# Block sums multiplied and copied beside a pair's own first scores, exponentials signalled one by one, and four weight loads queued last, in an attention and two-MoE kernel

## The reference

```python
k_sum = k.reshape(B, H, nb, block, D).max(axis=3)
v_sum = v.reshape(B, H, nb, block, D).mean(axis=3)
scores_l = scale * np.matmul(q, k.transpose(0, 1, 3, 2))
scores_s = scale * np.einsum('bhsd,bhnd->bhsn', q, k_sum) + np.log(block)
scores_all = np.concatenate([np.where(mask_l, scores_l, -1e9), scores_s], axis=-1)
a = softmax(scores_all)
out = np.matmul(a, np.concatenate([v, v_sum], axis=2))
```

## Time and profile before

| | |
|---|---|
| median of 3 runs | 379.94 us (379.44 to 381.62) |
| the profiled execution, its own time | 379.92 us |
| its span, first to last instruction | 378.2 us |
| PE, DVE, ACT, POOL busy | 86%, 47%, 38%, 27% of the span |
| mean granted TensorE clock | 0.969 of full |
| attention, soft mixture, switch layer | to about 122, to about 199, to the end |

### The profile page before, as it was taken

How to read it: one execution, slowest core, us unless ns; L and a number is a source line. 1 busy time by engine, 2 the same in 40 slices (tenths; PEclk the granted TensorE clock), 3 DMA queues, 4 the chain that set the end, 5 groups by cost and what they waited for, 6 DMA issues and landing times.

```text
span 378.2 us, 9016 instructions
## 1 busy us (share of the span) xinstructions
PE 326.6 (86%) x3272; PEld 233.9 (62%) x3273; DVE 175.9 (47%) x406; ACT 143.6 (38%) x329; POOL 101.1 (27%) x181
## 2 busy tenths in 40 slices
PE   0879879889898999969877795999999999999991
PEld 0556656667677754232325264788888888888880
DVE  2577867877885553360116596132331323213231
ACT  1476666666876422310110262123232322313221
POOL 5665675676764000000000000121211212112121
PEclk9999999999999999987998999699999999999996
DMA  7999999999999716999942900110101111010110
GB/s 306 362 425 408 414 423 415 419 419 420 410 385 406 297 50 227 383 390 405 393 156 83 364 2 0 57 47 36 55 28 55 41 42 55 28 55 34 49 56 32
DMA packets 23851, 81.64 MB, mean 216 GB/s; under 512 B 2312, under 2 KB 2312, under 8 KB 21776
## 3 DMA queue, kind: packets, MB, share of 16 engines
q1 hardware_dynamic: 20640, 73.08, 49.1%
q0 software_dynamic: 1920, 6.29, 4.4%
q10 hardware_dynamic: 1264, 1.92, 1.5%
HBM read 74.99 MB, written 6.29 MB: 215 GB/s over the span
## 4 chain that ended last, share of the span: by engine, by line
PE 57%; DMA 16%; DVE 11%; ACT 4%; POOL 4%; issue 4%; SPq 2%; ACTq 0%; DVEq 0%; POOLq 0%
PE ps L904 33%; DMA ring<-in_vt 11%; DMA ring<-in_moe_w 5%; PE ps L630 3%; POOL ring L503 3%; PE ps L643 3%; PE ps L890 3%; PE ps L600 3%; ACT work L962 2%; PE ps L787 2%; SPq L285 2%; PE ps L746 2%; DVE ps L1128 2%; PE ps L651 1%; PE ps L709 1%
## 5 line engine op out<-in xcount | busy, mean ns | idle before, releaser
L904 PE MATMUL ps<-high_w2b,hid_high 128*128 (+1 forms) x184 | 73.1, 397 | 4.1 <-DVE hid_low L1372 4.1
L904 PE MATMUL ps<-low_w2b,hid_high 128*128 (+1 forms) x184 | 72.8, 396 | 0.0
L904 PE MATMUL ps<-high_w2b,hid_low 128*128 (+1 forms) x184 | 72.5, 394 | 0.0
L962 ACT ACTIVATE work<-ps,small 128x120 f32<-128x120 f32 x192 | 53.9, 368 | 39.3 <-DVE small L1132 39.1
L556 POOL DMA_INDIRECT out_x<-work,small x24 | 23.6, 982 | 150.2 <-DVE small L1365 61.5
L1372 DVE SCALAR_TENSOR_TENSOR hid_low<-ps,hid_high 128x1024 fp32r<-128x1024 f32 x26 | 31.8, 1225 | 57.3 <-ACT hid_high L1062 57.3
L1044 ACT ACTIVATE work<-ps,small 128x512 f32<-128x512 f32 x24 | 16.5, 689 | 99.0 <-PE ps L904 99.0
L904 PEld LDWEIGHTS ps<-high_w2b,hid_high 128*128 128x128 f32 x184 | 35.3, 192 | 11.6 <-issue 4.5
L600 PE MATMUL ps<-ident,work 128*120 128x128 f32 x192 | 31.8, 289 | 10.8 <-ACT work L962 10.6
L904 PEld LDWEIGHTS ps<-high_w2b,hid_low 128*128 128x128 f32 x184 | 35.2, 191 | 7.5
L904 PEld LDWEIGHTS ps<-low_w2b,hid_high 128*128 128x128 f32 x184 | 35.3, 192 | 7.0
(11 more groups left out here) (230 smaller groups left out, 368.7 us busy)
## 6 DMA issues: line engine op xcount, KB each, us to landing
ring<-in_moe_w SPq DMA_DIRECT2D x13, 2048.0 KB, 13.4
ring<-in_qk SPq DMA_DIRECT2D x16, 1104.0 KB, 14.5
ring<-in_v SPq DMA_DIRECT2D x16, 780.0 KB, 10.1
ring<-in_moe_w SPq DMA_DIRECT2D x10, 512.0 KB, 11.3
ring<-in_vt SPq DMA_DIRECT2D x7, 384.0 KB, 8.8
comb<-in_vt SPq DMA_DIRECT2D x7, 384.0 KB, 8.2
x_or_g<-in_moe_w SPq DMA_DIRECT2D x1, 2048.0 KB, 9.0
whole_w2b<-in_moe_w SPq DMA_DIRECT2D x4, 512.0 KB, 9.0
```

What stands on the lines that cost most here:

```text
L904: last = pe.matmul(ps[:, 4 + u, :], hidden_part[:, u, m * P:(m + 1) * P], matrix[:, bass.ds(e * UNIT + m * DM, DM)], start=m == 0 and i == ...
L962: last = act.activation(probs[u][:, j, :], sc[u][:, j // 2, (j % 2) * KC:(j % 2 + 1) * KC], ACT.Exp, bias=negmax[u][:, j:j + 1], scale=flo ...
```

## The change

Five edits. (1) The PSUM place of the block sums moves from the bank of the value product to the bank of the scores. (2) PE issues the matmul for the sums of pair n inside `scores` of the pair's own first step, behind the waits for `gaps_filled` and `vb_ready`; for pair 0 little changes. (3) The copy to `vsum` moves from DVE to ACT, behind the four exponentials of the pair's first step, and waits there also for `sums_filled` of the pair before. (4) Each exponential signals `exp_done` by itself, and each of the four transposes waits for its own. (5) All four early units are issued behind the last v. Pair 0 keeps a copy on DVE with a semaphore of its own, and POOL does fill_sums(0) ahead of halve(1).

```diff
-    EARLY_BEHIND = ((1, 1), (2, 1), (3, 3), (3, 3))
+    EARLY_BEHIND = ((3, 3),) * 4
...
             def fill_sums(n):
-                pool.wait_ge(vsum_ready, n + 1)
+                if n:
+                    pool.wait_ge(vsum_ready, n)
+                else:
+                    pool.wait_ge(first_vsum, 1)
...
             fill_gaps(0)
+            fill_sums(0)
             halve(1)
-            fill_sums(0)
...
             def scores(b, s):
                 if g == 0:
                     pe.wait_ge(gaps_filled, b * NPAIR + pair + 1)
                     pe.sem_inc(pair_started, 1)
+                    if not (isinstance(b, int) and b * NPAIR + pair == 0):
+                        pe.wait_ge(vb_ready, b * NPAIR + pair)
+                        sums_by_block(block_sums[u], pair)
...
             def probs_T(b, s):
-                pe.wait_ge(exp_done, b * NSTEP + s + 1)
                 for j in range(4):
+                    pe.wait_ge(exp_done, (b * NSTEP + s) * 4 + j + 1)
...
             def weighted_values(b, s):
-                if g == 0:
-                    ahead_pair(sums_by_block, b, pair + 1, u)
...
             def exps(b, s):
-                last.then_inc(exp_done, 1)
+                                   bias=...).then_inc(exp_done, 1)
+                if s % NG == 0 and not (isinstance(b, int) and b * NSTEP + s == 0):
+                    n = b * NPAIR + s // NG
+                    act.wait_ge(vsum_done, n + 1)
+                    act.wait_ge(sums_filled, n)
+                    act.activation(vsum[3 * SLAB:4 * SLAB, 1:1 + P], block_sums[u], ACT.Copy).then_inc(vsum_ready, 1)
...
             def attended(b, s):
-                if g == 0:
-                    ahead_pair(copy_block_sums, b, pair + 1, u)
```

More of the change, by code:

```diff
@@ L200, in attention_soft_moe_switch_moe @@
         av = [flat[:, (6 + u) * BANK:(7 + u) * BANK] for u in range(2)]
-        block_sums = [av[u][3 * SLAB:4 * SLAB, BANK - P:BANK] for u in range(2)]
+        first_sums = av[0][3 * SLAB:4 * SLAB, BANK - P:BANK]
+        block_sums = [flat[3 * SLAB:4 * SLAB, 2 * u * BANK + BANK // 2:2 * u * BANK + BANK // 2 + P] for u in range(2)]
         disp_T = [ps[:, 2 + u, 0:S // 2] for u in range(2)]
@@ L222, in attention_soft_moe_switch_moe @@
         vT_loaded = [sem(f"vT_loaded{u}") for u in range(2)]; vb_ready = sem("vb_ready"); first_vb = sem("first_vb")
-        vsum_done = sem("vsum_done"); vsum_ready = sem("vsum_ready"); sums_filled = sem("sums_filled")
+        vsum_done = sem("vsum_done"); vsum_ready = sem("vsum_ready"); first_vsum = sem("first_vsum"); sums_filled = sem("sums_filled")
         kmax_ready = sem("kmax_ready"); gaps_filled = sem("gaps_filled"); pair_started = sem("pair_started"); top_seq = sem("top_seq")
@@ L572, in _, with sums_by_block @@
             pe.wait_ge(consts_ready, 1)
+            def sums_by_block(to, pair):
+                pe.matmul(to, vb[pair % 2], ident[:, :], start=True, stop=True, tile_position=(0, 3 * SLAB),
+                          skip_group_check=True).then_inc(vsum_done, 1)
             def scores(b, s):
@@ L665, in _ @@
             scores(0, 0)
-            sums_by_block(0, 0, 0)
+            pe.wait_ge(first_vb, 1)
+            sums_by_block(first_sums, 0)
             scores(0, 1)
@@ L961, in exps @@
                 for j in range(4):
-                    last = act.activation(probs[u][:, j, :], sc[u][:, j // 2, (j % 2) * KC:(j % 2 + 1) * KC], ACT.Exp,
-                                          bias=negmax[u][:, j:j + 1], scale=float(D) ** -0.5)
-                last.then_inc(exp_done, 1)
+                    act.activation(probs[u][:, j, :], sc[u][:, j // 2, (j % 2) * KC:(j % 2 + 1) * KC], ACT.Exp,
+                                   bias=negmax[u][:, j:j + 1], scale=float(D) ** -0.5).then_inc(exp_done, 1)
+                if s % NG == 0 and not (isinstance(b, int) and b * NSTEP + s == 0):
[3 more added lines that the diff above has]
+                    act.activation(vsum[3 * SLAB:4 * SLAB, 1:1 + P], block_sums[u], ACT.Copy).then_inc(vsum_ready, 1)
             def batch(b, last_batch):
@@ L1141, in halve_first @@
                 dve.tensor_tensor(vb[0][:, 0:NB], t[:, 0:NB], t[:, NB:2 * NB], ALU.add).then_inc(first_vb, 1)
[L1143 to L1151, removed]
             def attended(b, s):
@@ L1183, in _ @@
             row_max(0, 0)
-            copy_block_sums(0, 0, 0)
+            dve.wait_ge(vsum_done, 1)
+            dve.tensor_copy(vsum[3 * SLAB:4 * SLAB, 1:1 + P], first_sums).then_inc(first_vsum, 1)
             row_max(0, 1)
```

## The result

The changed kernel takes 404.58 us (median of 5 runs, 403.64 to 408.11) against 379.83 us before: a ratio of 1.0661, 95% interval 1.0607 to 1.0716. It is slower by 24.8 us, where 22.0 were forecast (401.9, range 398 to 410). The profiled execution is the slowest of the five, 408.11 us; four of them lie between 403.6 and 405.8.

The account below looks back on a forecast made before the run. The prediction read GpSimd as the old beat and a loop through four engines as the new bound: 21.9 us for 13 pairs plus 1.1 at the start, less 1.0 at the tail, made 379.9 + 22.0 = 401.9 us, range 398 to 410.

Parts of the forecast that it names:

- The loop: Attention, each pair: gaps to scores, exponentials, ACT's copy and back to GpSimd, 8.43 us against 6.75, 21.9 us more.
- The copy: In the pair's loop: ACT's 32x128 copy of the block sums, taken as 0.30 us, between 0.25 and 0.61.
- the step before it: In the pair's loop, ahead of ACT's copy: four exponentials until ACT's next instruction, 0.99 us.
- Start and tail: Attention's ends: gaps of pair 2 at 24.48 us, adding 1.1; behind the last gaps 1.0 us given back.
- The rival of the clock: Attention: TensorE's clock falls at times in the loop's waits, 404 to 415 us; chance 0.18.
- TensorE's 1 us in the relay: In the pair's loop: block sums, mask and scores, 1.03 us, growing by up to 0.9 at low clock.
- the estimate in the prediction: Attention: if matmuls restart slow after the wait in every turn, the kernel is at 415 us or beyond.
- The faster rival: Attention: the loop does not bind, pairs fall near TensorE's 6.0 us, 10 us less, 370 us; chance 0.05.
- the beat of the kernel before: Attention before the change: GpSimd nearly full and strictly serial, its fills 6.63 us apart, 1.76 us of that idle.
- that cover: Attention: the loop leaves TensorE 2 us to spare a pair, so shorter waits for exponentials gain nothing there.
- the stalls: Attention: GpSimd's waits for a late vT, 0.12 us a pair in the mean, go away with the early units moved.

Follow-up runs that it names:

- Experiment 4: Kernel before with only the block sums' matmul and copy moved (early units and exponential signals as before): 404.33 us, ratio 1.0635.
- Experiment 5: Changed kernel with halve(n+1) ahead of fill_sums(n) in GpSimd's program: 380.25 us, ratio 0.9999.
- experiment 6: Changed kernel with ScalarE's copy of the block sums ahead of the four exponentials, still behind the row maximum: 388.61 us, ratio 1.0208.
- Experiment 10: Kernel before with single exponential signals, all four early units last, and halve(n+1) ahead of fill_sums(n): 379.59 us, ratio 0.9988.
- experiment 12: Kernel of Experiment 10 with DVE's copy of the block sums moved behind the next row maximum: 378.33 us, ratio 0.9951.
- experiment 1: Changed kernel with the early units back in their old places: 404.72 us, ratio 1.0635.
- experiment 2: Kernel before with only single exponential signals and a wait of each transpose for its own: 378.67 us, ratio 0.9953.
- experiment 7: Changed kernel with eight extra 128x128 products on TensorE ahead of each wait for the gaps but the first: 403.29 us, ratio 1.061.

## Why the prediction was right

**The loop.** It was worked out as 3.57 + 4.86 = 8.43 us and measured 3.67 + 4.87 = 8.54 at full clock. The copy was priced at 0.30 and takes 0.27; an estimate by the Trainium skill (ScalarE: Activation LUTs, What ACT_TABLE_LOAD costs) was 0.29, and the trace agrees within 0.02. What was short is the step before it: I took 0.99 us from the first exponential to the next instruction, and the copy came after 1.14, since it did not start ahead of the last exponential's end. Experiment 4 has the whole loss without edits 4 and 5. Experiments 5 and 6 shorten the loop in two places, and the pair follows: 8.54, then 7.54 with the exponentials out of the loop, and 6.55, with GpSimd no longer in the chain, when halving is out of it. So the mechanism is shown, not only argued.

**Start and tail.** The gaps of pair 2 ended at 24.59 (forecast 24.48). Behind the last gaps (139.12) the attention took 10.74 us more; before it was 122.55 - 111.05 = 11.50. That gives back 0.8 where 1.0 was forecast. vT held no halving up: each fill from pair 1 on is followed by its halving within 0.1 us.

**Where the 2.7 us come from.** Of the difference between the median and 401.9, 13 x 0.11 = 1.4 us is the longer loop. The sum had no term for the time outside the span, which is 2.2 us in the execution of 404.58 us and was 1.7 before: 0.5. The later start (0.1) and the smaller gain at the tail (0.2) are the rest of what can be named. What remains, 0.5 us, is less than the stages behind the attention vary by, so it can't be given to the clock or to anything else. In the profiled, slowest execution the clock can be seen: 13 x (8.81 - 8.54) = 3.5 us lie in pairs longer than 8.54, and at 87 to 90 us it was at 0.50. In the profile of experiment 4, an execution of 404.05 us, 14 pairs took 8.59 us in the mean.

**The rival of the clock** was half right. It falls, in some pairs, as feared. But the loop's own slack takes most of that up, since only TensorE's 1 us in the relay counts, and the 404 to 415 given for it were too dear: the slowest execution, at 408, is in it, the median at its lower edge. The Trainium skill (TensorE: Matmul & The Clock Gate, HAM oscillation — how this bites in real kernels) describes a kernel in which the matmuls restart at the low clock after the wait in every turn; the waits of that kernel are longer than the 2 us here, which the prediction passed over. Had it been so here, the kernel would have been at 415 by the estimate in the prediction. Here about half the pairs even of the slowest execution keep 8.53 to 8.67 us, so a wait of this size alone does not bring the low clock each time.

**The faster rival** is refuted as forecast, but its price was wrong too. I had a pair fall to TensorE's 6.0 us once the loop did not bind, 370 us. Experiment 5 opens the loop and gets 6.55 us, 380. The step that failed is the sentence in which I read GpSimd as the beat of the kernel before, because it was nearly full. I also wrote that the chain that ended last goes through GpSimd in every pair. It does so only up to 78.2 us, around the loads of vT that are waited for: a halving frees a buffer, a vT is loaded into it, a later halving takes it up (loads from 35.60 for 12.36 us and from 63.63 for 11.59). From there on the chain of the kernel before has no GpSimd in it:

```profile
91.94 0.64 PE ps L630 x16
...
92.69 0.30 DVE vsum L1145
...
93.69 0.67 DVE ps L1128
...
94.83 0.87 ACT work L962 x3
...
95.75 0.65 PE ps L600 x4
...
98.57 0.64 PE ps L630 x16
```

These are the 6.63 us of a pair (98.57 less 91.94), and scores began 1.15 us after their gaps were full, so GpSimd had room. Experiment 10 agrees: it takes halving out of the way and the pair stays at 6.54. What held it was the round of value product, DVE's copy, division, row maximum, exponentials, transposes and their copy, in which GpSimd is not; it is read from the two chains, and experiment 12 moves it by 0.07 us a pair only.

**Edit 4** was costed at nothing while the loop binds, and 0.6 us a pair without that cover. The first is borne out (experiments 1 and 4 agree). The second was too much: experiment 2 got 0.1 us a pair.

**Edit 5** was put at nothing beyond the stalls. In the changed kernel it is nothing; alone on the kernel before it gives 2.2 us by the medians. The two pairs with a stall (2.13 and 1.35 us long) had taken 8.12 and 7.35 us from fill to fill instead of 6.63, since the next wait for DVE's copy was shorter behind each: 2.2 us together. Behind the attention TensorE waited for units for 1.3 us at L783 and 3.6 at L850, against 0.7 and 3.9 for the same work before, so the late units cost nothing that can be told from noise.

## What to carry to other kernels

When a producer's step is moved behind a consumer's, write down the loop that it closes before pricing the step: here moving a copy of 0.3 us cost 25 us, because it made an engine's 4.9 us of serial work wait for the scores that waited for that work. An engine that is nearly full is not thereby the bound; only what the chain passes through is. Read the chain over several pairs and in more than one part of the stage, and then swap the order of that engine's own program: that tests it for the price of two lines. The swap also cured the loop here (experiment 5): it does, ahead of the wait, all the work of that engine that doesn't need it. It has a price of its own where that work waits for a load, 3.5 us in experiment 10.

## What the hardware showed that was not expected

The clock fell after a stretch like that from 84 to 87 us, and only in some of the pairs, though all run the same program. TensorE's wait that ended at 86.38 was 1.93 us long, and the clock was low behind it; the next, at 95.17, was 0.93, since the work before it had run slowly, and the clock stayed at 1.00 from 96 to 99 us. In the kernel before the clock stayed at 1.00 from 24 to 110 us, the stretch at 48 us with 1.60 of 3 us busy included. Eight products of no use, which kept TensorE busy for 1.84 us from 91.79, held it at 1.00 from 24 to 110 us without lengthening a pair. A single wait of 2.41 us near the start was enough in experiment 10 for some 6 us at 0.50.

Executions of the changed kernel spread more than those of experiment 7: 403.64 to 408.11 against 402.92 to 403.87. That the clock is the reason is likely and wasn't tried apart; it is a comparison of five executions with four.
